# Fused linear attention and two expert layers on one core: whole score products, another order of ScalarE's copies, and the last wait on GpSimd

## The chip, the cores and the metric

The kernel runs on one core of one Trainium2 chip. The time is that of one execution on the device, in microseconds; several executions are made and the median is given. A profile is taken of one execution; its span runs from the first to the last recorded instruction.

## What is computed

Three stages, all in float32. A linear attention with decay w and bonus u, for 2 batches, 8 heads, 768 tokens and 48 channels a head:

```
for t in range(S):
    kt, vt, rt = k[:, :, t], v[:, :, t], r[:, :, t]
    cur = einsum('bhd,bhe->bhde', u * kt, vt)
    y[:, :, t] = einsum('bhd,bhde->bhe', rt, state + cur)
    state = w[..., None] * state + einsum('bhd,bhe->bhde', kt, vt)
```

Its output, as 1536 rows of 384, goes through a feed-forward layer of width 2048 with a leaky rectifier (`g = max(h, 0) + alpha * min(h, 0)`), and that output through a layer of 8 experts of width 1024 with 384 slots each: each row goes to its best expert, is weighted by that expert's softmax probability, and written back to its place.

## The kernel before

**Tiles.** Attention goes by chunks of 128 tokens: T = 12 chunks, six (CT) for each batch. Heads lie in pairs, each head padded to 64 partitions, so four pairs (PAIRS) hold all eight. In a chunk, k_hat and r_hat are k and r scaled by powers of the decay, channels on partitions. The feed-forward layer takes 4 groups of 384 rows, then come the experts one after the other. In both, float32 products are made of three float32r products (high by high, high by low, low by high). Those stages are almost all TensorE matmuls of 384 columns, and they follow attention on TensorE with no barrier between.

**Engines.** The program is five instruction streams written out by hand, with semaphores between them; the order on an engine is the order in the code. In the attention stage, for chunk t:

- GpSimd makes k_hat, rw (r with the bonus) and r_hat, ahead of the others.
- TensorE: `k_turn(t+2)` transposes k_hat into the bank misc; `scored(t+1)` makes the scores k_hat by r_hat into two banks, one for each head of the pairs (h2); `stage2(t)` adds the state by r_hat (L1111, in chunks that are not a batch's first) and the masked scores by v (L1119) into y; `update(t+1)` is kn by v (L1096), the new part of the state. A semaphore follows each.
- ScalarE: `diagonals(t)` writes eight scaled identities into the buffer scores (L611); `kn_copy(t)` copies misc out as kn (L603); `x_high(t)` copies y(t) out as its high part (L618); in four chunks `split_high` converts a weight chunk (L594).
- VectorE: `mask(t)` copies the scores over the diagonals where a later token looks at an earlier one (L826, after diagonals(t) and scored(t)); `new_state(t)`; `x_low(t-1)`; `bonus_sums(t+2)`, which multiplies misc by rw (ruk, L812) and sums it to the factors of the diagonals (L818).

So misc has two readers in each chunk, kn_copy on ScalarE and bonus_sums on VectorE, one after the other. Before, bonus_sums reads first (except for t under 2) and kn_copy waits for it; k_turn of the next chunk waits for both.

**Tile shapes on TensorE.** A matmul whose weights have 64 rows or 64 columns uses a part of the array. In the trace the shape stands as rows*columns of the array: k_turn is 128*128, scored and the state product 64*64, the products L1119 and L1096 128*64.

**The end.** For each expert, `y_copy` on ScalarE (L727) weighs three tiles of 128 rows and GpSimd scatters them to the output (L566). The last three scatters count on the semaphore s_last, the others on s_out. After its last instruction each engine has a drain (it waits until its work is done) and then a barrier of all engines; these stand at line L160 in the trace.

Of the kernel before, what the change touches and what calls it, by code (L numbers as in the profile page):

```python
# [3 lines left out]
P = 128  # L4


def attention_moe_kernel(nc, att_rk, att_v, decay, bonus, chunks, alpha, w_gate, out, disp,
# [152 lines left out]
    with ctx:  # L160
# [105 lines left out]
        def a_bank(t, h2):  # L266
            return bank[2 * (t % 2) + h2]
# [60 lines left out]
        def _(sp):  # L328
# [102 lines left out]
                    load_w2(e, f)  # L431

            sp.wait_ge(s_out, 16 * GT * (E - 1))
            sp.wait_ge(s_last, 16 * GT)


        @block.gpsimd
        def _(pool):
# [140 lines left out]
            for i in reversed(range(GT)):  # L579
                y_scatter(E - 1, i, s_last)  # L580


        @block.scalar
        def _(act):
# [11 lines left out]
            def kn_copy(t):  # L596

                act.wait_ge(s_kt, t + 1)
                if t:
                    act.wait_ge(s_ruk, t + 1)  # L600

                reuse(act, s_s1, updates(max(t - 1, 0)))
                act.activation(kn[:, t % 2, :], misc[:, :], ACT.Copy).then_inc(s_kn, 1)  # L603
# [11 lines left out]
            def x_high(t):  # L615

                act.wait_ge(s_y, t + 1)
                act.activation(xh[:, :, t * P:(t + 1) * P], y_bank(t)[:, :].rearrange("p (a n) -> p a n", a=PAIRS),  # L618
                               ACT.Copy).then_inc(s_xh, 1)
# [3 lines left out]
            kn_copy(0)  # L623
            diagonals(0)
            for t in range(T):
                if t + 1 < T:
                    diagonals(t + 1)
                if t + 2 < T:
                    kn_copy(t + 2)
                x_high(t)  # L630
                if CT <= t < CT + EARLY:
                    split_high(t - CT)

            def g_high(g, f):
                s = g * NF + f
# [124 lines left out]
        def _(dve):  # L760
# [44 lines left out]

            def bonus_sums(t):

                if t < 2:
                    dve.wait_ge(s_kn, t + 1)
                dve.wait_ge(s_kt, t + 1)  # L810
                dve.wait_ge(s_rw, t + 1)
                dve.tensor_tensor(ruk[:, t % 2, :].rearrange("p (h n) -> p h n", n=D),  # L812
                                  misc[:, :].rearrange("p (h n) -> p h n", h=H)[:, :, 0:D],
                                  rw[:, t % 2, :].rearrange("p (h n) -> p h n", n=D), ALU.mult).then_inc(s_ruk, 1)
                dve.wait_ge(s_ruk, t + 1)

                reuse(dve, s_dg, t - 1)
                dve.tensor_reduce(diag[:, t % 2, :], ruk[:, t % 2, :].rearrange("p (h d) -> p h d", d=D),  # L818
                                  AX.X, ALU.add).then_inc(s_bon, 1)
# [227 lines left out]
        def _(pe):  # L1047
# [14 lines left out]
            def k_turn(t):  # L1062

                pe.wait_ge(s_khat, t + 1)

                reuse(pe, s_ruk, t)
                reuse(pe, s_kn, t)
                for a in range(PAIRS):
                    last = pe.transpose(misc[:, a * P:(a + 1) * P], k_hat[:, t % 3, a, :], ident[:, :])  # L1069
                last.then_inc(s_kt, 1)  # L1070

            def scored(t):

                pe.wait_ge(s_khat, t + 1)
                pe.wait_ge(s_rhat, t + 1)

                reuse(pe, s_masked, t - 1)
                for a in range(PAIRS):
                    for half in range(2):
                        for h2 in range(2):  # L1080
                            p = slice(h2 * HALF, (h2 + 1) * HALF)
                            tokens = slice(half * HALF, (half + 1) * HALF)
                            last = mm(a_bank(t, h2)[tokens, a * P:(a + 1) * P], k_hat[p, t % 3, a, tokens],  # L1083
                                      r_hat[p, t % RH, a, :], start=True, stop=True)
                last.then_inc(s_a, 1)

            def update(t):
# [316 lines left out]
```

## Time and profile before

| | us |
|---|---|
| median of 3 executions | 450.64 |
| lowest, highest | 448.54, 451.07 |
| the profiled execution, its own time | 451.07 |
| its span | 449.2 |
| TensorE busy | 423.4 |

The profile page lists busy time by engine (PE is TensorE, DVE VectorE, ACT ScalarE, POOL GpSimd, SP the engine that issues transfers), the span in slices, the chain of work that ended last and the costliest groups. PEld is the load of weights, which runs beside the matmuls. A name with q (POOLq) is the engine's sequencer: waits, branches, drains. The trace gives the same execution instruction by instruction; matmuls overlap, so the length of a block of them is read from its start to the start of the next. TensorE's granted clock is 1.00 at 2.4 GHz and 0.5 at 1.2.

### The profile page before, as it was taken

The numbers are of one execution on the slowest core, as the hardware profiler recorded it, in microseconds if no ns is written. First come the engines' busy times: TensorE is split into PE (matmuls) and PEld (weight loads), VectorE is DVE, ScalarE is ACT, GpSimd is POOL, SyncE is SP. The second block draws the span as 40 slices with busy tenths as digits, with TensorE's granted clock in tenths as the row PEclk, the third lists the DMA queues.
The fourth block names the chain that finished last, engine by engine and source line by source line (L and its number), as shares of the span: only waits on it lengthen the run. The fifth ranks groups of instructions, "written<-read, shape, count | busy, mean of one in ns | idle before, by whom it ended". The sixth has DMA issues, their size and how long they took to land.

```text
span 449.2 us, 9383 instructions
## 1 busy us (share of the span) xinstructions
PE 423.4 (94%) x3333; PEld 409.6 (91%) x3333; DVE 259.4 (58%) x555; ACT 197.1 (44%) x450; POOL 176.4 (39%) x189
## 2 busy tenths in 40 slices
PE   6799999999999999999999986699999999998893
PEld 5688889999999999999999985599999999998893
DVE  6798867775435333633437663444578684648820
ACT  2789943432311122111323332334568684548721
POOL 4999616553323532244535851420110311011112
PEclk9899999999999999999999998989999999999997
DMA  7996034537950000000013440683676866564000
GB/s 251 403 337 193 3 112 141 154 88 254 367 217 19 35 1 0 0 35 18 0 35 91 139 140 17 227 307 92 207 218 197 262 190 204 158 211 110 10 19 7
DMA packets 33935, 61.45 MB, mean 137 GB/s; under 512 B 4654, under 2 KB 26910, under 8 KB 33888
## 3 DMA queue, kind: packets, MB, share of 16 engines
q1 hardware_dynamic: 31008, 55.53, 38.4%
q0 software_dynamic: 2880, 5.29, 3.4%
q8 instruction: 29, 0.48, 0.4%
q14 instruction: 18, 0.15, 0.1%
HBM read 47.53 MB, written 14.79 MB: 139 GB/s over the span
## 4 chain that ended last, share of the span: by engine, by line
PE 79%; DVE 7%; ACT 5%; issue 3%; POOL 2%; DMA 2%; POOLq 0%; SPq 0%; DVEq 0%; ACTq 0%
PE bank L1150 20%; PE bank L1165 19%; PE bank L1275 18%; PE bank L1304 14%; ACT scores L611 3%; PE bank L1262 2%; PE bank L1119 1%; PE bank L1083 1%; ACT w_high L594 1%; DVE scores L826 1%; DMA xe<-routed_rows 1%; DVE neg L884 1%; DVE act_full L890 1%; PE bank L1111 1%; PE bank L1069 1%
## 5 line engine op out<-in xcount | busy, mean ns | idle before, releaser
L510 POOL TENSOR_TENSOR g_low<-act_full,g_high 128x384 fp32r<-128x384 f32 x63 | 63.8, 1012 | 114.5 <-ACT g_high L640 114.5
L640 ACT ACTIVATE g_high<-act_full 128x384 fp32r<-128x384 f32 x64 | 33.7, 526 | 150.0 <-DVE act_full L890 137.3
L1150 PE MATMUL bank<-x_split,w_high 128*128 (+1 forms) x384 | 98.4, 337 | 0.0
L884 DVE TENSOR_SCALAR neg<-bank,alpha_sb 128x384 f32<-128x384 f32 x64 | 39.2, 613 | 71.5 <-PE bank L1150 71.4
L566 POOL DMA_INDIRECT out<-y_out,token x24 | 25.2, 1049 | 124.6 <-ACT y_out L727 123.4
L1150 PEld LDWEIGHTS bank<-x_split,w_high 128*128 128x128 f32 x384 | 69.0, 188 | 0.2 <-issue 0.2
L1165 PE MATMUL bank<-w_high,g_high 128*128 128x384 f32 x189 | 65.1, 344 | 1.2 <-POOL g_low L510 1.2
L1150 PE MATMUL bank<-x_split,w_low 128*128 (+1 forms) x192 | 64.4, 336 | 0.0
L1165 PE MATMUL bank<-w_high,g_low 128*128 128x384 f32 x189 | 63.8, 337 | 0.0
L1165 PE MATMUL bank<-w_low,g_high 128*128 128x384 f32 x189 | 63.7, 337 | 0.0
L1275 PE MATMUL bank<-xe_high,w_high 128*128 128x256 f32 (+1 forms) x192 | 58.8, 306 | 1.6 <-DVE xe_low L1003 1.6
L1275 PE MATMUL bank<-xe_high,w_low 128*128 128x256 f32 (+1 forms) x192 | 57.4, 299 | 0.0
L1275 PE MATMUL bank<-xe_low,w_high 128*128 128x256 f32 (+1 forms) x192 | 57.3, 299 | 0.0
L983 DVE SCALAR_TENSOR_TENSOR expert_g_low<-bank,expert_g_high 128x256 fp32r<-128x256 f32 (+1 forms) x64 | 29.3, 458 | 43.7 <-ACT expert_g_high L694 41.0
L803 DVE TENSOR_TENSOR w_low<-w_raw,w_high 128x384 fp32r<-128x384 f32 x44 | 31.2, 717 | 28.1 <-ACT w_high L594 22.4
L1304 PE MATMUL bank<-w_high,expert_g_high 128*128 128x384 f32 x120 | 40.8, 340 | 2.3 <-DVE xe_low L1003 2.3
L1304 PE MATMUL bank<-w_low,expert_g_high 128*128 128x384 f32 x120 | 40.2, 335 | 0.0
L1304 PE MATMUL bank<-w_high,expert_g_low 128*128 128x384 f32 x120 | 40.1, 334 | 0.0
L694 ACT ACTIVATE expert_g_high<-bank 128x256 fp32r<-128x256 f32 (+1 forms) x64 | 26.3, 411 | 31.2 <-PE bank L1275 31.2
L1165 PEld LDWEIGHTS bank<-w_high,g_high 128*128 128x128 f32 x189 | 35.4, 187 | 3.6 <-POOL g_low L510 2.5
L1275 PEld LDWEIGHTS bank<-xe_high,w_high 128*128 128x128 f32 x192 | 37.0, 193 | 1.8 <-issue 1.8
L1275 PEld LDWEIGHTS bank<-xe_low,w_high 128*128 128x128 f32 x192 | 37.1, 193 | 0.0
(127 smaller groups left out, 796.2 us busy)
## 6 DMA issues: line engine op xcount, KB each, us to landing
w_raw<-chunks SPq DMA_DIRECT2D x96, 192.0 KB, 3.3
w_raw<-chunks SPq DMA_DIRECT2D x32, 384.0 KB, 3.2
rk_in<-att_rk SPq DMA_DIRECT2D x12, 704.0 KB, 6.3
routed_rows<-fill SPq DMA_DIRECT2D x1, 5211.0 KB, 17.3
xe<-routed_rows SPq DMA_DIRECT2D x7, 579.0 KB, 5.5
v_in<-att_v SPq DMA_DIRECT2D x12, 200.0 KB, 5.5
out<-fill SPq DMA_DIRECT2D x1, 2304.0 KB, 23.4
x_split<-x_split POOLq DMA_DIRECT2D x18, 48.0 KB, 2.6
```

The source lines that it names most:

```text
L510: pool.tensor_tensor(gl[:, f % 4, :], act_full[:, f % 2, :], gh[:, f % 4, :].bitcast(f32), ALU.subtract).then_inc(s_gl, 1)
L566: pool.indirect_dma_start(out=out, out_offset=bass.IndirectOffsetOnAxis(ap=token[:, e % 2, i:i + 1], axis=0), in_=y_out[:, e % 2, i, :], i ...
L611: last = act.activation(scores[:, t % 2, h % 2, h // 2, :], ident[:, :], ACT.Copy, scale=diag[:, t % 2, h:h + 1])
L640: act.activation(gh[:, f % 4, :], act_full[:, f % 2, :], ACT.Copy).then_inc(s_gh, 1)
L694: act.activation(egh[:, f, 0:n], bank[f % 4][:, 0:n], ACT.Relu).then_inc(s_mgh, 1)
L803: dve.tensor_tensor(wl[:, slot, part], raw[:, m, part], wh[:, slot, part].bitcast(f32), ALU.subtract).then_inc(s_wl1 if first else s_wl2, 1)
L884: dve.tensor_scalar(neg[:, f % 2, :], h, 0.0, alpha_sb[:, f:f + 1], ALU.min, ALU.mult)\
L983: dve.scalar_tensor_tensor(egl[:, f, 0:n], bank[f % 4][:, 0:n], 0.0, egh[:, f, 0:n].bitcast(f32), ALU.max, ALU.subtract).then_inc(s_mgl, 1)
L1150: last = mm(bank[f % 4][:, 0:G], a[:, f, w], x[:, kc, bass.ds(g * G, G)], start=kc == 0 and i == 0, stop=kc == KC - 1 and i == 2)
L1165: last = mm(bank[4 + i][:, 0:DM], a[:, f % 4, i * P:(i + 1) * P], w[:, slot, W1:CW], start=f == 0 and m == 0, stop=f == n - 1 and m == 2)
L1275: last = mm(bank[f % 4][:, 0:n], a[:, slot, w], x[:, e % 2, kc, 0:n], start=kc == 0 and i == 0, stop=kc == KC - 1 and i == 2)
L1304: last = mm(bank[4 + i][:, 0:DM], a[:, f, i * P:(i + 1) * P], w[:, s % SLOTS, W1:CW], start=f == 0 and m == 0, stop=f == NFE - 1 and m == 2)
```

## The change

Three edits. (1) `scored` makes each head's scores in one product of 64 rows by 128 columns of weights, where two products of 64 by 64 stood. (2) ScalarE's order in the chunk loop becomes x_high(t-1), kn_copy(t+2), diagonals(t+1); kn_copy no longer waits for bonus_sums, bonus_sums waits for kn_copy in every chunk, and k_turn waits for bonus_sums alone. (3) The wait for the last three scatters moves from SP to GpSimd.

```diff
@@ block.sync, end
             sp.wait_ge(s_out, 16 * GT * (E - 1))
-            sp.wait_ge(s_last, 16 * GT)
@@ block.gpsimd, end
             for i in reversed(range(GT)):
                 y_scatter(E - 1, i, s_last)
+            pool.wait_ge(s_last, GT * 16)
@@ block.scalar, kn_copy
                 act.wait_ge(s_kt, t + 1)
-                if t:
-                    act.wait_ge(s_ruk, t + 1)
@@ block.scalar, chunk loop
             for t in range(T):
+                if t:
+                    x_high(t - 1)
+                if t + 2 < T:
+                    kn_copy(t + 2)
                 if t + 1 < T:
                     diagonals(t + 1)
-                if t + 2 < T:
-                    kn_copy(t + 2)
-                x_high(t)
                 if CT <= t < CT + EARLY:
                     split_high(t - CT)
+            x_high(T - 1)
@@ block.vector, bonus_sums
-                if t < 2:
-                    dve.wait_ge(s_kn, t + 1)
-                dve.wait_ge(s_kt, t + 1)
+                dve.wait_ge(s_kn, t + 1)
@@ block.tensor, k_turn
                 reuse(pe, s_ruk, t)
-                reuse(pe, s_kn, t)
@@ block.tensor, scored
                 for a in range(PAIRS):
-                    for half in range(2):
-                        for h2 in range(2):
-                            p = slice(h2 * HALF, (h2 + 1) * HALF)
-                            tokens = slice(half * HALF, (half + 1) * HALF)
-                            last = mm(a_bank(t, h2)[tokens, a * P:(a + 1) * P], k_hat[p, t % 3, a, tokens],
-                                      r_hat[p, t % RH, a, :], start=True, stop=True)
+                    for h2 in range(2):
+                        p = slice(h2 * HALF, (h2 + 1) * HALF)
+                        last = mm(a_bank(t, h2)[:, a * P:(a + 1) * P], k_hat[p, t % 3, a, :],
+                                  r_hat[p, t % RH, a, :], start=True, stop=True)
```

On ScalarE, the start of the chunk loop, chunks 0 to 2, before (scores is the buffer of the diagonals, bank is misc for kn and y for x_split):

```order
6 L611 ACTIVATE scores<-ident,diag 128x128 [waits bonus_sums_ready]
7 L611 ACTIVATE scores<-ident,diag 128x128 x7
8 L603 ACTIVATE kn<-bank 128x512 [waits update_done,ruk_ready,k_hat_transposed]
9 L618 ACTIVATE x_split<-bank 128x4x128 [waits y_done]
10 L611 ACTIVATE scores<-ident,diag 128x128 [waits y_done,bonus_sums_ready]
11 L611 ACTIVATE scores<-ident,diag 128x128 x7
12 L603 ACTIVATE kn<-bank 128x512 [waits update_done,ruk_ready,k_hat_transposed]
13 L618 ACTIVATE x_split<-bank 128x4x128 [waits y_done]
```

The same place after:

```order
6 L602 ACTIVATE kn<-bank 128x512 [waits update_done,k_hat_transposed]
7 L610 ACTIVATE scores<-ident,diag 128x128 [waits bonus_sums_ready]
8 L610 ACTIVATE scores<-ident,diag 128x128 x7
9 L617 ACTIVATE x_split<-bank 128x4x128 [waits y_done]
10 L602 ACTIVATE kn<-bank 128x512 [waits update_done,k_hat_transposed]
11 L610 ACTIVATE scores<-ident,diag 128x128 [waits y_done,bonus_sums_ready]
12 L610 ACTIVATE scores<-ident,diag 128x128 x7
```

The copy to kn has moved ahead of the eight diagonal writes, and the copy of y stands one chunk later in the loop.

On TensorE, chunk 1 before (k_turn(3), scored(2), the state and v products of stage2(1), update(2)):

```order
10 L1069 MATMUL bank<-ident,k_hat 128x128 x4
11 L1083 MATMUL bank<-r_hat,k_hat 64x128 x16
12 L1111 MATMUL bank<-r_hat,state 64x128 x8
13 L1119 MATMUL bank<-scores,v_in 64x128 x8
14 L1096 MATMUL bank<-v_in,kn 64x48 x8
```

And after:

```order
10 L1067 MATMUL bank<-ident,k_hat 128x128 x4
11 L1079 MATMUL bank<-r_hat,k_hat 128x128 x8
12 L1107 MATMUL bank<-r_hat,state 64x128 x8
13 L1115 MATMUL bank<-scores,v_in 64x128 x8
14 L1092 MATMUL bank<-v_in,kn 64x48 x8
```

The scores block has half as many matmuls with outputs of all 128 partitions; the block behind it keeps its shape.

## Rows read from the trace of the kernel before

**Rows 1.** The page, part 1: busy us, share of the span, instructions.
```profile
PE 423.4 (94%) x3333; PEld 409.6 (91%) x3333; DVE 259.4 (58%) x555; ACT 197.1 (44%) x450; POOL 176.4 (39%) x189
```

**Rows 2.** Busy time by stretch: stretch, length, then engines, granted clock, DMA share, GB/s.
```profile
core 0: us, PE busy (x) PEld busy (x) DVE busy (x) ACT busy (x) POOL busy (x), PEclk, DMA share, GB/s
...
19.35:35.39 16.04, 16.04 (x332) 14.18 (x328) 14.90 (x29) 13.82 (x42) 16.04 (x14) 1.00 0.94 333
35.39:60.07 24.68, 23.52 (x498) 20.87 (x497) 20.84 (x40) 22.46 (x64) 16.81 (x16) 1.00 0.23 77
```

**Rows 3.** Timeline of TensorE in chunk 1: start us, us, instructions.
```profile
19.93 1.10 PE L1083 MATMUL bank<-r_hat,k_hat 64*64 64x128 f32 x32
20.86 1.05 PE L1111 MATMUL bank<-r_hat,state 64*64 64x128 f32 x16
21.84 1.09 PE L1119 MATMUL bank<-scores,v_in 128*64 128x128 f32 x16
22.77 0.62 PE L1096 MATMUL bank<-v_in,kn 128*64 128x48 f32 x16
```

**Rows 4.** Timeline of TensorE in chunks 4 to 6.
```profile
33.75 1.09 PE L1119 MATMUL bank<-scores,v_in 128*64 128x128 f32 x16
34.77 0.66 PE L1069 MATMUL bank<-ident,k_hat 128*128 128x128 f32 x4
...
37.27 1.09 PE L1119 MATMUL bank<-scores,v_in 128*64 128x128 f32 x16
...
38.74 0.66 PE L1069 MATMUL bank<-ident,k_hat 128*128 128x128 f32 x4
39.33 1.10 PE L1083 MATMUL bank<-r_hat,k_hat 64*64 64x128 f32 x32
40.36 1.09 PE L1119 MATMUL bank<-scores,v_in 128*64 128x128 f32 x16
```

**Rows 5.** Timeline of ScalarE in chunks 4 to 10.
```profile
34.89 0.60 ACT L618 ACTIVATE x_split<-bank 128x512 fp32r<-128x512 f32 x1 [0.56 <-PE bank L1119]
35.39 2.44 ACT L611 ACTIVATE scores<-ident,diag 128x128 f32<-128x128 f32 x8
...
38.41 0.60 ACT L618 ACTIVATE x_split<-bank 128x512 fp32r<-128x512 f32 x1
38.90 2.44 ACT L611 ACTIVATE scores<-ident,diag 128x128 f32<-128x128 f32 x8
41.24 0.58 ACT L603 ACTIVATE kn<-bank 128x512 f32<-128x512 f32 x1
41.72 0.59 ACT L618 ACTIVATE x_split<-bank 128x512 fp32r<-128x512 f32 x1
42.20 0.84 ACT L594 ACTIVATE w_high<-w_raw 128x768 fp32r<-128x768 f32 x1
42.93 2.45 ACT L611 ACTIVATE scores<-ident,diag 128x128 f32<-128x128 f32 x8
...
50.98 2.46 ACT L611 ACTIVATE scores<-ident,diag 128x128 f32<-128x128 f32 x8
...
55.01 2.46 ACT L611 ACTIVATE scores<-ident,diag 128x128 f32<-128x128 f32 x8
```

**Rows 6.** Timelines of VectorE and TensorE at the end of attention.
```profile
57.57 1.33 DVE L826 COPY_PREDICATED scores<-after,bank 128x512 f32<-128x512 int32 x2 [1.41 <-ACT scores L611]
...
59.05 1.09 PE L1119 MATMUL bank<-scores,v_in 128*64 128x128 f32 x16 [1.05 <-DVE scores L826]
60.07 0.62 PE L1150 MATMUL bank<-x_split,w_high 128*128 128x384 f32 x2
```

**Rows 7.** The end: GpSimd's timeline, then L434 and L160, durations in ns.
```profile
443.48 0.97 POOL L566 DMA_INDIRECT out<-y_out,token x1 [1.69 <-ACT y_out L727]
...
L434 SPq EVENT_SEMAPHORE  x1: 17/17/17, 445.9 to 445.9; - x1
...
L160 PEldq DRAIN  x1: 2700/2700/2700, 439.3 to 439.3; - x1
...
L160 POOLq DRAIN  x1: 5682/5682/5682, 443.3 to 443.3; - x1
```

## The prediction

> **What bounds the kernel now.** I read the page's busy times first. TensorE is busy for 94% of the span [rows 1], so nothing gets much faster unless TensorE waits somewhere. The table by stages [rows 2] then says where it does. From 19.35 to 35.39 us it is busy for all 16.04 us at the full clock (2.4 GHz, granted 1.00); from 35.39 to 60.07 us it lacks 1.2 us, and ScalarE has 22.5 of 24.7 us. So the attention stage has two halves: TensorE sets the pace in the first, ScalarE in the second. The timeline of TensorE [rows 3, 4] gives the length of each block of matmuls, from its start to the next block's start. The timeline of ScalarE [rows 5] shows a queue with hardly a gap from 34.89 us on, which repeats every 4.03 us (diagonals at 42.93, 50.98, 55.01: two periods of 4.03, then one). It ends in the diagonals of chunk 11 at 55.01 us; mask(11) on VectorE follows at 57.57 after 1.41 us of waiting for them, the last scores product at 59.05 after TensorE waited 1.05 us, and the first matmul of the feed-forward stage at 60.07 [rows 6]. From there TensorE has no long wait for this stage's work, so I carry a shift of the 60.07 through to the end at full size. At the other end of the program, the last row scatter starts at 443.48 us and has landed when SP's wait at L434 passes, at 445.9; the span lasts to 449.2. What lasts that long is GpSimd's drain at the block's end: 5.68 us from 443.3, so to 449.0 [rows 7].
>
> **Part 1: scores in one piece (L1076 to L1085).** Sixteen products of 64x64 weights a chunk become eight of 64x128. Both read 64 rows; the new form fills all 128 output partitions at once. The hardware runs each as two instructions. Before, 32 instructions on 128 columns take 0.93 us to the next block [rows 3]; the 16 of the scores-by-v product, which is 128 rows by 64 columns and goes two abreast, take 0.93 as well. So 64x64 goes four abreast, and 64x128 should go two abreast in the same 0.93: half the instructions, each twice as wide. I take the products themselves at no change. No row shows 64x128. If it went faster, the bound is that of fewer weight loads, which already hide under the matmuls; if one at a time, about 0.9 us more a chunk (a rival below).
>
> What does change is the shape's neighbours. The state product L1111 that follows is 64x64 too, so today there is no change of shape between them. Blocks of about equal work show what a change costs. Entered from another shape but left into the same one, the scores block takes 0.93 (19.93 to 20.86); with a change on both sides it takes 1.03 (39.33 to 40.36) [rows 3, 4]. The state block, changed only on leaving, takes 0.98; the block L1119 with a change on both sides takes 1.02 (33.75 to 34.77) against 0.93 with one on entry only [rows 3, 4]. So leaving costs 0.10 and entering 0.05: **0.15 us for each new change of shape**. There is one wherever scored(t+1) is followed by the state part of stage2(t): t = 1 to 5 and 7 to 10, nine times. The bounds are 0 (the change from 64x128 to 64x64 alters the columns only; the rows I have alter the rows, or both) and 0.15; I take 0.15, since all shape changes in the stage are followed by such a gap.
>
> The Trainium skill, TensorEngine Tiling (Array Packing), Key Properties, says that a change of tiling mode, as against a change of tile, drains TensorE, and it makes no exception for a change in columns alone. The trace shows the gap where both differ; by that rule the nine changes all cost it, and without it part 1 would be nothing.
>
> **Part 2: ScalarE's order (L622 to L632), with the waits that go with it.** Before: diagonals(t+1), kn_copy(t+2), x_high(t). After: x_high(t-1), kn_copy(t+2), diagonals(t+1). kn_copy(t+2) needs k_turn(t+2), which TensorE starts only after y(t-1) and an update. So ScalarE, which used to have ready diagonals to write in that time, now stands. Behind the waiting kn_copy are queued the diagonals, and behind those mask and the scores product. Also VectorE's ruk now waits for kn_copy instead of the other way round, and k_turn(t+1) for ruk.
>
> While TensorE sets the pace this costs nothing: y(t-1) to the end of k_turn(t+2) is about 1.1 us, then kn_copy 0.48, diagonals 2.34 [rows 5] and mask 1.4, some 5.3 us. The block L1119 starts every 3.97 us today (21.84 to 33.75 is three of them [rows 3, 4]) and every 4.12 with the new change; from the end of one, 1.09 after its start, to the start of the next but one are 7.1 us. VectorE has 14.90 busy of 16.04 us [rows 2], and a 4.12 us chunk leaves it more room. That is the cover, some 1.8 us.
>
> It costs in the second half, where ScalarE is the bound. I walk its queue from x_high(4), 34.89 before [rows 5]. Pitches, start to start, are x_high 0.50 (0.48 at 41.72), diagonals 2.34, kn_copy 0.48, weight copy 0.73. Four shape changes of 0.15 lie ahead of y(4), so x_high(4) starts at 35.49 and ScalarE is free at 35.99. k_turn(7), at 34.77 before, starts at 35.37, ends 0.66 later: kn_copy(7) at 36.07. Diagonals(6) 36.55, free at 38.89. y(5): the block at 37.27 moves by five changes to 38.02 and ends 1.09 later: x_high(5) at 39.16, a gap of 0.27, free at 39.65. k_turn(8), at 38.74 before [rows 4], is at 39.49 and done at 40.15: kn_copy(8) at 40.20, a gap of 0.55. Diagonals(7) 40.68 to 43.02, weight copy to 43.75. From here everything is there early and the queue runs full: x_high and kn_copy 0.96, diagonals(8) 44.71, (9) 48.74, (10) 52.77; then 2.34, a weight copy of 0.74 and x_high 0.48: diagonals(11) at 56.33, where it is 55.01 now. **Attention ends 1.32 us later.** With free shape changes the same walk gives x_high(4) 34.89, kn_copy(7) 35.48, x_high(5) 38.41, kn_copy(8) 39.45, diagonals(11) 55.58: +0.57. So the order alone is worth 0.57 and the shapes 0.75. The waits that were dropped (kn_copy for ruk, k_turn for kn) buy nothing: before, ruk was done long before kn_copy's turn came.
>
> **Part 3: the last wait, from SP to GpSimd (L434, L580).** Behind GpSimd's wait is queued only its drain; SP now ends early, which nobody needs. Before, the drain ran alongside the transfer. TensorE's drain ends with its last matmul (439.3 + 2.7 = 442.0 [rows 7], where the chain has the last product end). GpSimd's ends 4.5 us after its last descriptor work (443.48 + 0.97 = 444.45) and 3.0 us after the landing. What those 4.5 us are, the trace doesn't say. Three readings, with the wait passing at 445.9 and 0.2 us for the barrier. (a) They are the drain's own work after a scatter, whatever has landed: it starts at 445.9 and the span ends at 450.6, **+1.5 us**. (b) 3.0 us of work follow a landing: no change. (c) The drain only watches an unfinished transfer, slowly: it ends at once, the span at 446.2, -3.0 us. If all 5.68 us of it came after the wait the end would be 451.8, +2.6, the upper bound. I take (a): the drain's end has no visible tie to the landing, and a wait ahead of a fixed task only adds.
>
> **Sum.** The profiled execution took 451.07 us with a span of 449.2, so 1.9 lie around it. 449.2 + 1.3 + 1.5 + 1.9 = 453.9. That execution was 0.4 above the median of the three, 450.64; the forecast of a median is **453.5 us**, 0.6% slower. The three runs span 2.5 us, and a measurement of this kernel tells about 0.5%, 2.3 us, from no change; the forecast lies just beyond that.
>
> **Rivals.**
> - *The drain is short once the rows have landed* (reading c). For it: TensorE's drain ends with its last work. Against: GpSimd's went on 3.0 us beyond the landing. It decides once the drain after the wait takes under 1.8 us: the end then comes 1.3 us or more earlier against the wait's start, which pays for the attention stage. 450.64 + 1.3 - 3.0 = 448.9 us: not slower, nearly faster. Chance 0.23.
> - *The end does not move* (reading b): 450.64 + 1.3 = 452.0. Chance 0.18.
> - *The shape change is free*, with the drain as in (a): 450.64 + 0.6 + 1.5 = 452.7. For it: only columns change. Chance 0.12.
> - *64x128 products go one at a time.* Against it: four 64x64 already run together, two of them on the same columns. Ten blocks between 19.35 and the end by 0.9, less the 1.05 us that TensorE waits today, and the changes: about +9.5, and +1.5: 461.6. Chance 0.06.
> - *The forecast*: 0.37. What is left (0.04) is a wait that I missed.
>
> **How the numbers follow.** Of the forecast's 0.37, about 0.27 stays beyond 0.5% given the spread of runs; with some of the free-change case (0.05), the unmoved end (0.04) and the serial case (0.06) that makes slower 0.42. Faster needs the short drain and a lucky median: 0.07. The rest, 0.51, is within 0.5%. The likeliest single case lies beyond the line and the sum of the others within it. The range goes from the short drain (448.9, less 0.2) to the forecast with the drain's upper bound and some spread, 455.0; it leaves out the serial case and tails, under 0.2.
>
> **What would show it.** In the profile after: diagonals(11) near 56.3 and the first feed-forward matmul near 61.4; ScalarE idle before kn_copy in the chunks up to 8; the scores block at 1.03 us and the state block at 1.03; TensorE still at 2.4 GHz there. GpSimd's drain begins near 447.3 (445.9 + 1.3) and lasts 4.5 us under (a), 3.0 under (b), near nothing under (c). I am wrong if the scores block takes 1.8 us, if the chunk stays at 3.97, or if the drain ends with the landing.

## The result and the profile after

The changed kernel takes 455.83 us in the median (454.17 to 456.08), the kernel before on the same chip 450.08 (448.54 to 451.07): a ratio of 1.0122, 95% interval 1.0084 to 1.0163. Every ratio here is taken over the executions within 1.5% of the fastest of their kernel, while the medians and spreads beside it are of all executions, so a ratio isn't the quotient of two medians. The changed kernel is slower by more than was forecast (453.5 us), and the time is above the forecast's range (455.0). The profiled execution of the changed kernel took 453.51 us, span 451.8, so it was quicker than the four that were timed; before had 451.07, the slowest of its four, and 449.2 us. The 2.6 us between the two spans are therefore not the whole difference, and the experiments below had to find the rest.

First the blocks of TensorE in chunks 1 and 2, which answer to [rows 3] (start us, us, instructions):

```profile
20.13 1.16 PE L1079 MATMUL bank<-r_hat,k_hat 64*128 64x128 f32 x16
21.23 1.09 PE L1107 MATMUL bank<-r_hat,state 64*64 64x128 f32 x16
22.25 1.09 PE L1115 MATMUL bank<-scores,v_in 128*64 128x128 f32 x16
23.17 0.62 PE L1092 MATMUL bank<-v_in,kn 128*64 128x48 f32 x16
23.72 0.66 PE L1067 MATMUL bank<-ident,k_hat 128*128 128x128 f32 x4
24.31 1.16 PE L1079 MATMUL bank<-r_hat,k_hat 64*128 64x128 f32 x16
...
40.55 1.16 PE L1079 MATMUL bank<-r_hat,k_hat 64*128 64x128 f32 x16
41.65 1.09 PE L1115 MATMUL bank<-scores,v_in 128*64 128x128 f32 x16
```

Start to start, the scores block now takes 1.10 us (0.93 before), the state block 1.02 (0.98), and a chunk 4.18 (20.13 to 24.31) instead of 3.97. The 16 instructions on 64*128 tiles run two abreast: one at a time would have been 1.8 us. The last two lines are scored(7), with the 128*64 products right behind it; it takes 1.10 us too. Next, ScalarE in chunks 4 to 11, which answers to [rows 5]:

```profile
31.73 0.60 ACT L617 ACTIVATE x_split<-bank 128x512 fp32r<-128x512 f32 x1 [0.22 <-PE bank L1115]
32.76 0.60 ACT L602 ACTIVATE kn<-bank 128x512 f32<-128x512 f32 x1 [0.43 <-PE bank L1067]
...
35.91 0.60 ACT L617 ACTIVATE x_split<-bank 128x512 fp32r<-128x512 f32 x1 [0.22 <-PE bank L1115]
...
39.63 0.60 ACT L617 ACTIVATE x_split<-bank 128x512 fp32r<-128x512 f32 x1 [0.22 <-PE bank L1115]
40.66 0.60 ACT L602 ACTIVATE kn<-bank 128x512 f32<-128x512 f32 x1 [0.43 <-PE bank L1067]
41.15 2.44 ACT L610 ACTIVATE scores<-ident,diag 128x128 f32<-128x128 f32 x8
...
56.77 2.47 ACT L610 ACTIVATE scores<-ident,diag 128x128 f32<-128x128 f32 x8
```

ScalarE now stands 0.43 us for k_turn before kn_copy(6) at 32.76 and before kn_copy(8) at 40.66. From there on its queue runs without a gap to diagonals(11) at 56.77, which started at 55.01 before. The end of attention on TensorE, as [rows 6]:

```profile
60.82 1.09 PE L1115 MATMUL bank<-scores,v_in 128*64 128x128 f32 x16 [0.95 <-DVE scores L825]
61.84 0.44 PE L1146 MATMUL bank<-x_split,w_high 128*128 128x384 f32 x1
```

The feed-forward stage starts 1.77 us later. And the end of the program, as [rows 7] (GpSimd's timeline, then line 160, the drains at the block's end, in ns, with their starts):

```profile
444.48 0.97 POOL L565 DMA_INDIRECT out<-y_out,token  x1 [1.69 <-ACT y_out L728]
...
L160 SPq DRAIN  x1: 7/7/7, 435.9 to 435.9; - x1
...
L160 POOLq COMPARE_BRANCH  x1: 38/38/38, 446.9 to 446.9; - x1
L160 POOLq DRAIN  x1: 4475/4475/4475, 447.1 to 447.1; - x1
```

GpSimd's wait passes at 446.9, its drain then takes 4.48 us, and the span ends at 451.8. Before, the drain ran beside the transfer.

The table gives the stages of the traces that the text speaks of, in us: attention up to the start of the first feed-forward product, the feed-forward stage, the gate with the gathering of expert 0's rows, the experts (of these expert 0, and experts 1 to 3 together), and from the start of the last product to the end of the span. "Filled by 128" and "gaps filled" are versions that the experiments explain.

| kernel | attention | feed-forward | gate | experts | expert 0 | experts 1 to 3 | end |
|---|---|---|---|---|---|---|---|
| before | 60.07 | 210.96 | 19.95 | 150.67 | 27.68 | 53.83 | 7.53 |
| after | 61.84 | 211.06 | 18.91 | 150.83 | 26.09 | 55.74 | 9.15 |
| part 3 alone | 59.91 | 210.97 | 18.88 | 150.64 | 27.69 | 53.83 | 9.15 |
| part 1 alone, first | 62.07 | 210.99 | 20.19 | 152.82 | 28.75 | 55.07 | 7.53 |
| part 1 alone, third | 60.42 | 210.94 | 20.38 | 153.85 | 28.71 | 56.14 | 7.53 |
| part 2 alone | 61.28 | 210.99 | 19.74 | 150.60 | 27.66 | 53.83 | 7.53 |
| part 1, filled by 128 | 61.69 | 210.99 | 19.58 | 150.61 | 27.66 | 53.83 | 7.53 |
| before, filled by 128 | 59.06 | 211.25 | 19.58 | 152.56 | 27.65 | 55.89 | 7.53 |
| before, filled by 256 | 60.43 | 225.75 | 19.76 | 150.46 | 27.64 | 53.83 | 7.53 |
| after, filled by 128 | 62.05 | 210.99 | 19.73 | 148.91 | 26.09 | 53.83 | 9.15 |
| before, gaps filled | 59.11 | 210.98 | 19.53 | 148.91 | 26.09 | 53.83 | 7.53 |
| after, gaps filled | 61.14 | 211.04 | 19.21 | 149.01 | 26.07 | 53.83 | 9.15 |

Between before and after the table has +1.77 in attention, +0.10, -1.04 in the gate, -1.59 in expert 0, +1.91 in experts 1 to 3, -0.16 in the others, and +1.62 at the end. The first and the last of these were forecast; the two large ones in the experts were not. The gate's difference is within what two traces of one kernel show: three traces of the changed kernel have 18.9, 19.8 and 19.0 us, two of before 19.95 and 19.4.

### The profile page after: what moved, and what is told of

Read it like the earlier page. It is cut to its first block, busy times and chain, and to the rows that moved or that the text cites. A ratio compares the mean times of both kernels' runs of the same rounds, so it can differ in the third digit from the quotient of the medians.

```text
span 451.8 us, 8997 instructions
## 1 busy us (share of the span) xinstructions
PE 425.0 (94%) x3141; PEld 410.1 (91%) x3141; DVE 257.5 (57%) x555; ACT 197.8 (44%) x450; POOL 175.9 (39%) x189
## 4 chain that ended last, share of the span: by engine, by line
PE 80%; DVE 7%; ACT 5%; issue 3%; POOL 2%; DMA 0%; POOLq 0%; ACTq 0%; DVEq 0%
PE bank L1146 20%; PE bank L1161 19%; PE bank L1271 16%; PE bank L1300 14%; ACT scores L610 2%; PE bank L1052 2%; PE bank L1079 2%; PE bank L1115 2%; ACT w_high L595 1%; PE bank L1107 1%; PE bank L1258 1%; PE bank L1067 1%; DVE neg L883 1%; DVE act_full L889 1%; DVE xe_low L1002 1%
## 5 line engine op out<-in xcount | busy, mean ns | idle before, releaser
L889 DVE SCALAR_TENSOR_TENSOR act_full<-bank,neg 128x384 f32<-128x384 f32 x64 | 35.7, 557 | 2.4
```

The costliest lines, as they stand in the source:

```text
L889: dve.scalar_tensor_tensor(act_full[:, f % 2, :], h, 0.0, neg[:, f % 2, :], ALU.max, ALU.add)\
```

## The experiments

### Each part alone, and the whole again

Part 3 alone is the edit at L434 and L580, part 1 alone the new scored(), part 2 alone ScalarE's order with the waits that go with it, each as in the diff above.

> The kernel before with part 3 alone: GpSimd waits for the last three scatters, SP doesn't. Three small costs (the costs measured in the two profiles add up, and nothing else happens): GpSimd's drain takes 4.5 us and starts when the rows have landed, the span ends 1.5 to 1.6 us later, ratio about 1.0035; attention's first feed-forward matmul stays at 60.1 us. Something more: the runs of the changed kernel are 5.7 us above those of before, where the stages of its profile explain 3.4. If the missing 2.3 hang on this wait, this kernel is 3.9 us slower, ratio about 1.0085.

Measured: 451.88 us against 449.5, ratio 1.0038 (1.0018 to 1.0057). Attention, feed-forward stage and experts are those of before to 0.2 us, and the end is 9.15 us instead of 7.53: +1.62.

> The kernel before with part 1 alone: eight score products of 64 by 128. Three small costs: the scores block takes 1.10 us and the state block 1.02, the first feed-forward matmul comes at about 61.4 us (+1.3), ratio about 1.003. Something more: if the missing 2.3 us hang on the shape (a clock that is granted otherwise, in later stages too), this kernel is 3.6 us slower, ratio about 1.008.

Measured: 453.42 us, ratio 1.0071 (1.0045 to 1.0097), with executions from 451.6 up to 460.3. Attention's end and, unforeseen, the experts moved: 152.82 us against 150.67.

> The kernel before with part 2 alone: ScalarE's order and the waits that go with it, scores in 64 by 64. Three small costs: diagonals(11) at about 55.6 us, the first feed-forward matmul at 60.6 (+0.6), ratio about 1.001. Something more: if the missing 2.3 us hang on the order, 2.9 us slower, ratio about 1.0065.

Measured: 450.79 us, ratio 1.0018 (1.0002 to 1.0034). Attention ends at 61.28; the rest is as before.

> The changed kernel itself once more, beside its parts on one chip and with a second profile. Three small costs: its ratio is that of the three parts together, about 1.0075 (3.4 us), and the 1.012 of the first comparison was partly the spread of a few runs. Something more: about 1.012 again, and this profile shows in which stage after attention the 2.3 us lie, which the first profile doesn't (its later stages are 0.8 us shorter than before's).

Measured: 454.32 us, ratio 1.0108 (1.0071 to 1.0146).

So the largest single loss is the shape's, where the forecast had 0.75 us for it in attention. Four more runs, on another chip, asked whether that holds.

> The kernel before against itself, for the spread and for a second profile of it. Three small costs: ratio 1.000, first feed-forward matmul near 60 us; if the stretch at half clock (14.5 to 17.9 us in the first profile) falls elsewhere, that start moves by up to 1.2 us either way, since it is what differs most between the profiles of the four kernels so far (10.4, 14.8, 15.7 and 15.8 us, and none). Something more: the same.

Measured: 450.36 us against 449.75, ratio 0.9996 (0.9977 to 1.0015).

> Part 1 alone once more, with a second profile. It was 3.2 us slower in the median (1.0071, 1.0045 to 1.0097) where the blocks explain 1.3, with a longer upper tail (up to 460.3 us) than the kernel before (up to 451.5). Three small costs: ratio near 1.003 when repeated, later stages as in before. Something more: near 1.007 again, and in this profile the extra lies in stretches at half clock, in attention or where the experts begin (there it was 6.8 us at half clock in the first profile of this kernel, 3.4 in before).

Measured: 454.75 us, ratio 1.0118 (1.0081 to 1.0155).

> Part 1 alone a third time, for a third profile and more timings. Three small costs: as before but for 1.3 us, ratio 1.003. Something more: 1.007, and the same stage longer as in the other two profiles of this kernel.

Measured: 456.92 us (451.79 to 466.42), ratio 1.0099 (1.0059 to 1.0139). The experts take 153.85 us.

> The changed kernel a third time. Its two profiles have a span of 451.8 and 450.8 us though its median is 454.3 to 455.8. Three small costs: ratio 1.0075. Something more: 1.011, and if this profile falls on a long execution (span over 452.5) it shows which stage is long.

Measured: 455.25 us, ratio 1.0108 (1.0077 to 1.0139).

The loss repeats, and it comes with a wide spread of all executions: the three runs of the shape alone have executions up to 460.3, 458.2 and 466.4 us, where before stays under 451.6. One part of it sits in the same place in every trace. Experts 1, 2 and 3 take 17.95, 17.93 and 17.95 us in every trace so far without part 1, and up to 19.05 each in those with it (together 55.07 to 56.14 us instead of 53.83). In two of the three traces of part 1 alone expert 0 is 1.0 us longer as well (28.75 and 28.71); there the granted clock is at its lower level for 6.8 us where before has 3.4, so this share of the loss goes with the clock, and why the stretch is longer stays open. The experts' code doesn't differ at all. What does differ shows when TensorE's timeline is read where expert 2 goes from its up to its down products, in the changed kernel:

```profile
345.48 0.49 PE L1258 MATMUL bank<-ident,xe 128*128 128x128 f32 x3
346.86 0.41 PE L1300 MATMUL bank<-w_high,expert_g_high 128*128 128x384 f32 x1 [0.89 <-DVE expert_g_low L982]
```

and in the table of waits of 325 to 375 us (engine, line waited for: us, times, longest):

```profile
PEld bank L1300 <- issue: 1.9, 3, 1.1
PE bank L1300 <- DVE expert_g_low L982: 0.9, 1, 0.9
```

The same table of before has neither line. "Issue" is time in which nothing that the profile shows was waited for; the releaser of the second line is only the last semaphore. Between the two products lies a jump: experts that have at most 256 rows skip the other branch of the If. So I read the records of TensorE's sequencer on the line of that If (count, then shortest, median and longest in ns, first and last start). The one jump of expert 2, in before and in the changed kernel:

```profile
L1326 PEldq COMPARE_BRANCH  x1: 379/379/379, 344.3 to 344.3; - x1
```

```profile
L1322 PEldq COMPARE_BRANCH  x1: 2451/2451/2451, 343.9 to 343.9; - x1
```

It takes 2.45 us where it took 0.38. The sequencer runs ahead of the products and comes to it at 343.9, which hides a part; it ends at 346.35, and the first product behind it starts at 346.86. From 320 to 370 us, which covers experts 1 to 3, the same line reads, in before, in the changed kernel, and in the third run of part 1 alone:

```profile
L1326 PEldq COMPARE_BRANCH  x6: 70/343/383, 326.3 to 369.4; - x6
```

```profile
L1322 PEldq COMPARE_BRANCH  x5: 70/1673/2451, 325.6 to 362.9; - x5
```

```profile
L1324 PEldq COMPARE_BRANCH  x5: 70/1793/2292, 328.1 to 365.4; - x5
```

Section 3 of the page names a suspect, the queue that brings the program itself. Before and after:

```profile
q8 instruction: 29, 0.48, 0.4%
```

```profile
q8 instruction: 28, 0.46, 0.4%
```

That is one packet of 16.4 KB at a time. 0.4% of 16 engines over 449.2 us are 28.7 us, so some 1.0 us a packet. Part 1 takes 192 weight loads and 192 matmuls out of TensorE's program ahead of the experts, and everything behind lies elsewhere in those pieces.

The Trainium skill, Runtime: NRT & Kernel Launch, Instruction fetch mechanics, says that an engine's program comes in blocks of 16 KiB or 256 instructions, prefetched in sequence only, and that a taken branch whose target isn't in the current window waits for a fetch. The packets' size in the trace agrees, and so do the runs that follow, which were built on the number 256.

### Moving the program without changing the work

The filler is an instruction that adds 1 to a semaphore nobody reads, behind the first products of the feed-forward stage's first group:

```diff
@@ block.tensor, up() and products(), group 0 only
                         last = mm(bank[f % 4][:, 0:G], a[:, f, w], x[:, kc, bass.ds(g * G, G)],
                                   start=kc == 0 and i == 0, stop=kc == KC - 1 and i == 2)
+                        fill(g)      # shortened: pe.sem_inc(s_pad, 1), not behind a step's last product, until the count is there
```

> Part 1 alone (the new shape of the scores), and with it 128 instructions of TensorE's sequencer that do nothing but add 1 to a semaphore that nobody reads, one behind each of the first 128 products of the FFN's first group. They stand there because part 1 takes 96 products of the scores, in the trace 192 weight loads and 192 matmuls, out of TensorE's program, and the trace shows the program being fetched in pieces of 16 KB, 28 of them where before had 29. Theory A (place in the program): in every trace with part 1 so far the jump that ends the first branch of experts 1, 2 and 3 takes TensorE's sequencer 1.25 to 2.45 us, in every trace without it 0.37 to 0.38 us, because what it jumps to lies otherwise in those pieces. At 64 bytes an instruction (worked out: 175 instructions and 5.8 us between two pieces at a chunk of 3.97 us give 256 in a piece) 384 fewer shift the program by one piece and a half, and 128 more put it back on a whole number. So those jumps back at 0.37 us, the experts at 150.6 us instead of 152.5 to 153.9, and the ratio at 1.002 to 1.005 (what part 1 costs in attention, 1.1 to 1.4 us) instead of 1.007 to 1.012. Rival B (the later start of the experts, or other phases of the weight transfers, makes the loss): the 128 instructions change nothing of that, the jumps stay at 1.2 to 2.5 us, experts 152.5 or more, ratio 1.008 to 1.012. Rival C (the increments cost something of their own): the FFN stage, 210.96 us before, gets longer by up to 128 times 0.05 us.

Measured: 450.14 us against 449.45, ratio 1.0017 (0.9997 to 1.0038), no execution above 452.3.

> The kernel before with the same 128 increments and nothing else changed. Theory A: its program is now shifted by half a piece, as part 1 shifts it, so the loss comes without part 1: the jumps behind experts 1 to 3 at 1.2 to 2.5 us instead of 0.37, the experts at 152.3 to 153.9 us instead of 150.6, attention at 60 us as before, ratio 1.004 to 1.008. Rival B: nothing happens, ratio 1.000, jumps 0.37 us. Rival C: the FFN longer, the experts as before.

Measured: 452.11 us (450.89 to 461.4), ratio 1.0058 (1.0034 to 1.0082).

> The kernel before with 256 increments, two behind each product in the same place, a whole piece of 16 KB. Theory A: the jumps stay at 0.37 us and the experts at 150.6 us, ratio 1.000, although twice as many instructions were added as in the run beside it. Rival B: 1.000 as well. Rival C: the FFN is longer by twice what the 128 gave, ratio above that of the run with 128.

Measured: 463.76 us, ratio 1.0316 (1.0283 to 1.0348), all of it in the feed-forward stage, which takes 14.8 us more; the experts are those of before.

> The changed kernel, all three parts, with the 128 increments. Theory A: jumps at 0.37 us, experts 150.5 us or less, the end still 9.15 us; what is left is attention's +0.5 to +1.8 us and the end's +1.6 us: ratio 1.005 to 1.008 instead of 1.011. Rival B: 1.011 as it was.

Measured: 452.51 us, ratio 1.0057 (1.0037 to 1.0077).

The jumps of experts 1 to 3, in this order (part 1 filled by 128, before filled by 128, before filled by 256, after filled by 128):

```profile
L1338 PEldq COMPARE_BRANCH  x5: 70/367/398, 327.6 to 363.4; - x5
```

```profile
L1340 PEldq COMPARE_BRANCH  x5: 70/1812/2291, 325.2 to 362.7; - x5
```

```profile
L1340 PEldq COMPARE_BRANCH  x7: 70/318/383, 330.5 to 384.3; - x7
```

```profile
L1336 PEldq COMPARE_BRANCH  x6: 70/281/313, 326.5 to 369.6; - x6
```

The kernel before, with its work untouched, gets the loss from 128 idle instructions: experts 1 to 3 at 55.89 us instead of 53.83, and an execution of 461.4 us. With 256 it has none. Part 1 with the 128 loses it. A later start of the experts or other phases of the transfers (rival B) can't do that: filled by 256, before starts its experts 15 us later and keeps its quick jumps.

The packets of the instruction queue say what a slow jump waits for. In the twenty traces of this case 26 jumps of TensorE's sequencer take over 1 us, and each ends 1.33 to 1.51 us after a packet of 16.4 KB of that queue has ended. The slow jump of expert 2 above (343.9 to 346.35) has its packet from 343.5 to 344.9. The quick one of before, at 344.3, has none between 340.1 and 346.4. So the jump waits for a piece of the program that is still on its way, and it is as long as that piece is late.

By the ratios the position costs part 1 alone 0.5 to 1.0% (1.0071 to 1.0118 against 1.0017), 2.4 to 4.5 us, and the whole change 0.5 to 0.65% (1.0108, 1.0108 and 1.0122 against 1.0057), 2.3 to 2.9 us. The traces show 1.2 to 2.3 us of it in experts 1 to 3; the jumps' length differs between executions. None of the long executions (458 us and more) was profiled, so what makes them long isn't shown.

### The clock's two stretches, and a faster version

Two things were left. In the traces of the changed kernel, filled or not, expert 0 takes 26.1 us and 27.64 or more in all others so far. And attention ends about 1 us apart in executions of the same kernel. Both go with TensorE's clock. The busy table of before, 287 to 295 us and 8 to 18 us (length, PE, PEld, DVE, ACT, POOL, granted clock, DMA share, GB/s):

```profile
287.00:295.00 8.00, 5.26 (x24) 4.79 (x23) 4.89 (x9) 4.05 (x7) 3.95 (x3) 0.79 1.03 368
```

```profile
8.00:18.00 10.00, 6.20 (x97) 4.77 (x97) 7.14 (x14) 5.97 (x18) 9.13 (x8) 0.83 1.03 407
```

In both the granted clock drops to its lower level, 1.2 GHz, in a part of the time, behind idling: 1.58 us ahead of expert 0's first product, 1.44 and 2.36 us in the first two chunks. So transposes into free banks were put in:

```diff
@@ block.tensor, ahead of the experts
             for i in range(GT):
                 turn_xe(0, i, bank[4 + i])
+                if i == GT - 2:
+                    keep_warm(6)
+            keep_warm(12)
@@ block.tensor, start of attention (second version only)
             k_turn(0)
+            keep_warm(12, 4)
             scored(0)
             update(0)
             k_turn(1)
+            keep_warm(18, 4)
```

> The kernel before with 18 more transposes into a free bank: 6 behind the second tile of expert 0's rows, 12 behind the third, where TensorE stands for 1.2 us (the third tile's transfer) and 1.6 us (the split of the rows). In eight traces of kernels without all three parts the granted clock is halved for 3.4 or 6.8 us around 290 to 293 us, the first products of expert 0 take 0.52 us instead of 0.34, and expert 0 takes 27.65 to 28.75 us; in the four of the changed kernel and its filled variant this stretch is missing and expert 0 takes 26.1 us. Theory A (TensorE's idling there is what the clock answers): with the gaps filled the stretch goes, expert 0 at 26.1 us, ratio 0.996 to 0.998. Rival B (the clock there follows something else, as the drop behind the gate at 277 us, or the load on the chip): the stretch stays, 27.65 us, ratio 1.000. Rival C: the transposes come late and hold up the first product, ratio 1.001 to 1.003. The program is 36 instructions longer, a seventh of a piece of 16 KB: whether the jumps behind experts 1 to 3 stay at 0.37 us or not shows how near the edge the program stands.

Measured: 451.82 us, ratio 1.0045 (1.0022 to 1.0068). Slower, though the clock did what theory A says. TensorE's timeline and busy table at expert 0:

```profile
287.54 1.47 PE L1053 MATMUL bank<-ident 128*128 128x128 f32 x12
289.17 0.44 PE L1275 MATMUL bank<-xe_high,w_high 128*128 128x384 f32 x1 [0.15 <-issue]
```

```profile
287.00:295.00 8.00, 7.85 (x53) 7.59 (x52) 6.00 (x11) 4.47 (x8) 3.97 (x3) 1.00 1.00 338
```

Granted 1.00 throughout, and expert 0 takes 26.07 us. What ate it lies in experts 5, 6 and 7. The line of the second If, 400 to 440 us, reads here:

```profile
L1336 PEldq COMPARE_BRANCH  x6: 65/130/3092, 403.0 to 434.1; - x6
```

and in before:

```profile
L1333 PEldq COMPARE_BRANCH  x6: 65/127/190, 406.4 to 436.3; - x6
```

Thirty-six instructions, a seventh of a piece, were enough to make other jumps slow: two of this line, 3.09 and 2.45 us long, in experts 5 and 6, which take 16.21 and 15.57 us instead of 15.23 and 15.35. Expert 7 takes 14.25 us instead of 12.62 with no slow jump. There TensorE stands 1.45 us between two products of one step, which the profile puts down to issue, and goes on at 437.2, 1.37 us after an instruction packet has ended. So it seems that straight code can wait for its next piece too.

> As the run beside it, and with 12 transposes ahead of the first chunk's scores and 18 behind the second chunk's transposes, in gaps of 1.4 and 2.4 us of TensorE in the first 15 us, where in some executions the clock is halved for 3.4 us (at 14.5 us in the kernel before) and attention ends 1.0 us later (60.07 and 60.16 against 59.06 us where it isn't). 96 instructions more in all; 160 increments in the FFN's first group, one behind a product, fill them up to a whole piece, so the jumps stay at 0.37 us. Theory A: attention at 59.1 us in the trace, expert 0 at 26.1 us, FFN longer by up to 0.4 us, ratio 0.994 to 0.997. Rival B: nothing gained in either place, ratio 1.000 to 1.002 for the fill.

Measured: 448.04 us (447.61 to 448.5) against 450.15, ratio 0.9963 (0.9948 to 0.9978). Attention 59.11 us, expert 0 26.09, no jump above 0.38 us. The busy table of 8 to 18 us:

```profile
8.00:18.00 10.00, 9.26 (x154) 8.25 (x154) 8.00 (x16) 6.29 (x19) 9.14 (x8) 1.00 1.03 406
```

TensorE is kept at 2.4 GHz by 3 us more of work that nobody needs. This version beats both kernels, and its executions lie within 0.9 us. It is also filled by 160 increments to a whole piece.

> Parts 1 and 2 together, the end as before. Each part alone leaves expert 0 at 27.65 us or above, the three together give 26.1 us in four traces of four. If parts 1 and 2 are what moves the missing half-clock stretch, expert 0 is 26.1 us here, and the ratio is that of the whole change less the end's 1.6 us: 1.007 to 1.009. If it takes the end's part too, expert 0 is 27.65 us and the ratio 1.010 to 1.012. The jumps behind experts 1 to 3 take 1.2 to 2.5 us in both cases.

Measured: 453.2 us, ratio 1.0077 (1.005 to 1.0103). Expert 0 27.66 us, experts 1 to 3 55.94.

> Parts 2 and 3 together, the shape of the scores as before. The jumps behind experts 1 to 3 at 0.37 us (TensorE's program is as long as before), experts 1 to 3 at 17.95 us, the end 9.15 us instead of 7.53, attention 60.9 to 61.3 us. Ratio 1.004 to 1.006 if expert 0 is 27.65 us, 1.000 to 1.003 if it is 26.1 us.

Measured: 451.57 us, ratio 1.0036 (1.0019 to 1.0054). Expert 0 27.66 us, experts 1 to 3 53.83, the end 9.15, attention 60.93.

Neither pair brings the 26.1 us of the whole; parts 1 and 3 together weren't tried. TensorE idles as long ahead of expert 0 in the changed kernel, 1.69 us in its trace, so what spares it the lower clock stays open. For expert 0 the idling is needed: in the three traces of before with these gaps filled the drop is gone. It doesn't suffice, as the changed kernel shows. In attention the drop is absent from the three traces with filled gaps, but also from six of the seventeen without, so there the filling is less surely the cause.

> The changed kernel, all three parts, with the 48 transposes of the filled version of before in the same three gaps, and 32 increments in the FFN's first group, so that TensorE's program is shorter than before's by a whole piece of 16 KB (and one instruction). Both disturbances, the slow jumps and the half-clock stretches of attention and expert 0, are then out of both kernels, and what is left between this one and the filled before is what the three parts cost themselves. Theory: attention 60.4 to 60.7 us against 59.1 (the new shape and ScalarE's order, 1.3 to 1.6), the end 9.15 against 7.53, experts 148.9 both: 2.9 to 3.3 us above the filled before, that is 451.0 us, ratio 1.001 to 1.004 to before, 1.0065 to 1.0075 to the filled before. Rival: the parts cost less once the clock is whole (the shape's cost in attention was the clock's), ratio to the filled before 1.0036 to 1.005, the end's alone.

Measured: 451.12 us (450.8 to 451.48) against 449.4, ratio 1.0033 (1.0022 to 1.0044).

> The filled version of before once more, on the same chip as the filled version of the changed kernel. It gave 0.9963 to before (0.9948 to 0.9978): the same again, 0.995 to 0.998, attention 59.1 us, expert 0 26.1 us, jumps 0.3 us.

Measured: 447.93 us (447.66 to 448.06), ratio 0.9965 (0.9951 to 0.998).

With both disturbances out of both kernels, the change costs 451.12 - 447.93 = 3.19 us, and the traces say where: attention 61.14 against 59.36 (the second trace of the filled before; the first, in the table, has 59.11), the end 9.15 against 7.53, together 3.40 (the other stages differ by 0.01 in sum). The sum in the prediction had 2.8.

## Why the prediction was right, and where it was wrong

**What bounds the kernel.** Right: the second half of attention ran at ScalarE's pace, and the shift of its end was carried whole into the feed-forward stage, which took 210.96 and 211.06 us. Wrong was to take that as far as the end: gate and expert 0 gave back 2.6 us in the trace (the gate's 1.0 of it is spread between executions), and experts 1 to 3 took 1.9.

**Part 1, the products.** Right: 64x128 goes two abreast, and the rival of serial tiles (461.6 us) is out. **The shape change** was under-sized. The scores block with a change on both sides takes 1.10 us, not 1.03; the state block 1.02, against 1.03 forecast. So the new change costs 1.10 + 1.02 - 0.93 - 0.98 = 0.21 us, not 0.15. The excess sits in the scores block. Scored(7), which has the 128*64 products behind it, takes 1.10 us too (40.55 to 41.65), where the 64*64 block between two changes took 1.03. So leaving for 64*64, a change of columns alone, costs as much as leaving for 128*64, and the 0.07 more belong to the entry into 64*128 or to the pace of its products; which, isn't shown. The rival of a free change in the columns is out. The Trainium skill, TensorEngine Tiling (Array Packing), Key Properties, says that a change of tiling mode drains TensorE. The trace agrees, by these 0.21 us.

**Part 1, what was left out.** This is the step that failed. The sum held for part 1 only what happens where its products stand, and counted "half the instructions" as nothing but pace. It took 384 instructions out of a program that has jumps behind, and these were 1.3 to 2.1 us longer each in experts 1 to 3. By the ratios the whole change loses 2.3 to 2.9 us by its position. The forecast was a loss of 2.9 us (453.5 against 450.64) and the medians give 5.75 (455.83 against 450.08), so this one term about makes up what the forecast lacked. No rival named it; "a wait that I missed" had 0.04. The profile of before could have warned: it shows jumps of 0.38 us on L1326 where others take 0.07, and a queue that brings the program in 29 packets.

**Part 2.** The walk held step by step. It forecast gaps of ScalarE of 0.27 us before x_high(5) and 0.55 before kn_copy(8), a full queue from then on, and diagonals(11) at 56.33; the trace has 0.22, 0.43 and 56.77. The 0.44 us more are there at the walk's start: x_high(4) stands at 35.91 instead of 35.49. Four shape changes, each 0.06 dearer, make 0.24 of it, and 0.2 us chunk 1 was late already (20.13 against 19.93). Diagonals(7), at 41.15 against 40.68, shows it carried unchanged. Attention ended 1.77 us later, not 1.32. Both of these traces have a stretch at the lower clock in attention; where there is none, the changed kernel ends it at 60.6 us in two traces and before, filled by 128, at 59.1, a shift of 1.5. Alone, the order costs 0.8 us by its ratio (0.1 to 1.5), where the walk had 0.57; in its one trace attention ends 1.2 us later.

**Part 3.** Reading (a) was right, and (b) and (c) are out. The drain takes 4.48 us once the wait has passed, and in each trace with part 3 the end is 9.15 us, +1.62 where +1.5 was forecast. Part 3 alone measured +0.38%, 1.7 us.

**The sum.** The terms that it had came to 2.8 us, and their clean measure is 3.19 us. The median was missed because of a term that it didn't have. The 0.23 for reading (c) was much, for a trace in which the drain went on 3.0 us behind the landing; between (a) and (b) that trace could not decide. The range's upper end had the drain's upper bound in it and nothing for a later stage.

## What to carry to other kernels

A matmul saved on TensorE is also two or four instructions less in its program. If runtime branches follow, read the sequencer's records on their lines before and after: here each jump of over 1 us ended 1.3 to 1.5 us behind an instruction packet, and idle instructions in a place with slack made it quick again. Compare two variants of a kernel only at the same position of their jumps, or the position is measured instead of the edit. And where the granted clock drops behind a gap of TensorE ahead of a long dense stage (1.58 us here), filling the gap may be worth more than the rearrangement in question.

## What the runs showed of the hardware

- **Jumps of TensorE's sequencer** take 0.07 to 0.40 us, or 1.25 to 3.1 us, by where the program lies in pieces of 256 instructions: a shift by 128 or by 36 made some of them slow, a shift by 256 none. A slow one ends 1.33 to 1.51 us after an instruction packet has ended (26 of 26). Their length differs from execution to execution. The kernels with them reach 466.4 us, against a spread of 0.9 us in the version with quick jumps and a full clock; that the jumps make the longest executions isn't shown.
- **Semaphore increments on TensorE** are nearly free one at a time and not two at a time. With one behind each of 128 products the feed-forward stage took 210.99, 210.99 and 211.25 us in three traces (210.96 without); with two, 14.8 us (225.75), so 0.12 us for each product that is followed by two. The records show the same 51 ns for each:

```profile
L1145 PEldq EVENT_SEMAPHORE  x256: 51/51/51, 59.7 to 100.8; - x128
```

```profile
60.00:101.00 41.00, 40.96 (x154) 26.35 (x151) 21.76 (x38) 11.71 (x19) 14.65 (x22) 1.00 0.37 112
```

  The weight loads are busy for 26.4 of 41 us there, where the run with one increment has 24.92 of 26 (59 to 85 us). That the loads come too late there to hide under the products is a reading of this, not shown.
- **GpSimd's drain** behind scatters takes 4.48 us of its own, after the rows have landed, and without a wait ahead it ended 4.5 us after GpSimd's last scatter too. The wait is added at full size: the drain starts 1.6 us after the last scatter's own work (447.1 against 445.45), and the end is 1.62 us later.
